# Two staging slots instead of three, and another order of the first products, in a fused attention and feed-forward kernel

## The reference, cut to what matters

```python
# 4 batches, 8 heads, 576 tokens, head size 64; d_model 512, d_ff 1536 and 2048
kv  = einsum('bhsd,bhse->bhde', k, v)
out = einsum('bhsd,bhde->bhse', q, kv)
x   = out / sqrt(mean(out*out, axis=-1) + 1e-6) * g_norm      # then tokens x 512
g   = x @ w_gate                                              # layer 1
y   = (g * sigmoid(g) * (x @ w_val)) @ w_out
h   = y @ w_in2                                               # layer 2
out = (max(h, 0) + log1p(exp(-abs(h)))) @ w_out2
```

## Time and profile before

| what | value |
|---|---|
| median of 3 runs | 906.13 us (906.01 to 907.18) |
| profiled execution | 906.13 us |
| its span, first to last instruction | 904.3 us |
| PE busy | 896.2 us (99% of the span) |
| DVE, ACT, POOL busy | 527.7, 354.8, 80.0 us |
| mean granted TensorE clock | 0.999 |

### The profile page before, as it was taken

The page is one execution under the profiler, slowest core; times in us unless marked ns, Lnnn a source line. Parts: engine busy times, 40 slices in busy tenths (PEclk is TensorE's granted clock), DMA queues, the critical chain, the costliest instruction groups (busy, mean ns, idle before and its releaser), DMA issues.

```text
span 904.3 us, 13404 instructions
## 1 busy us (share of the span) xinstructions
PE 896.2 (99%) x5146; PEld 850.1 (94%) x5146; DVE 527.7 (58%) x1009; ACT 354.8 (39%) x615; POOL 80.0 (9%) x44
## 2 busy tenths in 40 slices
PE   8999999999999999999999999999999999999998
PEld 7999999999999999999999989998998998999987
DVE  3656642453254314224234888878878878878875
ACT  5616420342034201001232754554544644644553
POOL 4635000000000000000454000000000000000000
PEclk9999999999999999999999999999999999999999
DMA  9982342133111200000243000000000000000000
GB/s 277 215 208 82 87 77 54 47 93 71 53 37 45 73 1 1 1 1 1 71 138 119 1 1 1 35 0 0 35 0 0 35 0 0 35 0 0 36 1 35
DMA packets 81129, 44.38 MB, mean 49 GB/s; under 512 B 36672, under 2 KB 73664, under 8 KB 81088
## 3 DMA queue, kind: packets, MB, share of 16 engines
q1 hardware_dynamic: 80928, 43.80, 18.2%
q10 hardware_dynamic: 160, 0.00, 0.0%
HBM read 35.52 MB, written 8.26 MB: 48 GB/s over the span
## 4 chain that ended last, share of the span: by engine, by line
PE 98%; issue 0%; DMA 0%; DVE 0%; POOL 0%; ACT 0%; ACTq 0%; POOLq 0%; SPq 0%
PE bank L655 24%; PE bank L657 24%; PE bank L656 24%; PE bank L772 7%; PE bank L773 7%; PE bank L771 7%; PE bank L595 2%; PE bank L588 1%; PE bank L663 1%; PE bank L669 0%; PE bank L561 0%; DMA q<-in_q 0%; PE bank L578 0%; PE bank L550 0%; PE bank L571 0%
## 5 line engine op out<-in xcount | busy, mean ns | idle before, releaser
L655 PE MATMUL bank<-x_hi,arena 128*128 128x384 f32 x938 | 315.1, 336 | 0.0
L657 PE MATMUL bank<-x_hi,arena 128*128 128x384 f32 x938 | 314.6, 335 | 0.0
L656 PE MATMUL bank<-x_lo,arena 128*128 128x384 f32 x938 | 314.0, 335 | 0.0
L655 PEld LDWEIGHTS bank<-x_hi,arena 128*128 128x128 f32 x938 | 176.2, 188 | 4.4
L656 PEld LDWEIGHTS bank<-x_lo,arena 128*128 128x128 f32 x938 | 176.1, 188 | 3.8
L657 PEld LDWEIGHTS bank<-x_hi,arena 128*128 128x128 f32 x938 | 176.0, 188 | 0.0
L1114 DVE TENSOR_TENSOR act_a<-act_a,bank 128x384 f32<-128x384 f32 x72 | 39.9, 554 | 228.1 <-PE bank L657 225.1
L899 ACT ACTIVATE act_a<-bank 128x384 f32<-128x384 f32 x72 | 35.3, 491 | 244.2 <-PE bank L657 240.3
L919 ACT ACTIVATE act_a<-bank 128x384 f32<-128x384 f32 x96 | 47.3, 492 | 179.1 <-PE bank L657 179.1
L773 PE MATMUL bank<-arena,g_lo 128*128 128x512 f32 x288 | 113.8, 395 | 0.0
L772 PE MATMUL bank<-arena,g_hi 128*128 128x512 f32 x288 | 113.6, 395 | 0.0
(11 more groups left out here) (90 smaller groups left out, 838.7 us busy)
## 6 DMA issues: line engine op xcount, KB each, us to landing
stage<-in_moe_w_out SPq DMA_DIRECT2D x28, 256.0 KB, 3.6
out_dram<-out_stage SPq DMA_DIRECT2D x18, 256.0 KB, 2.0
k<-in_k SPq DMA_DIRECT2D x16, 256.0 KB, 3.2
v<-in_v SPq DMA_DIRECT2D x16, 256.0 KB, 3.2
stage<-in_moe_w_in SPq DMA_DIRECT2D x16, 256.0 KB, 2.8
xy<-in_q SPq DMA_DIRECT2D x48, 72.0 KB, 3.0
stage<-in_moe_w_gate SPq DMA_DIRECT2D x12, 256.0 KB, 3.8
stage<-in_moe_w_val SPq DMA_DIRECT2D x12, 256.0 KB, 4.1
```

Source lines behind the costliest of these rows:

```text
L655: nc.tensor.matmul(ps, hi, rhs_hi, start=first, stop=False)
L656: nc.tensor.matmul(ps, hi, rhs_lo, start=False, stop=False)
L657: return nc.tensor.matmul(ps, lo, rhs_hi, start=False, stop=last)
```

## The change: what it does

- `STAGE1` goes: two slots hold the raw weights of layer 1, so load f waits for `w_ready` of step f - 2, and not f - 3. Load 2 waits for step 0 and stands behind the wait for the first transposes; load 3 stands ahead of the eight DMAs of `next_pair`, not behind them.
- The semaphores of the two layers' staging are shared.
- In a round of the first attention q times kv comes ahead of the next transpose of q, and two idle products stand in each round behind the kv product.
- The transposed x of all four rounds goes to bank 7; each transpose of x but the first waits until the previous one has been split (`xs_ready`).
- On ACT `part_high(1, "gate")` comes behind the last `first_x_high`, and the table is loaded ahead of both.
- On ACT at k = 2, `split_high(4)` comes ahead of the two roots of the late tiles.

```diff
-IDLE_PRODUCTS = (7, 2)
-STAGE1 = 3
+IDLE_PRODUCTS = (7, 2, 2)
...
-    stage1 = sb("stage1", [P, STAGE1, RAW1], F32, over="xy", shift=4 * (TOKENS * KT - STAGE1 * RAW1))
+    stage1 = sb("stage1", [P, 2, RAW1], F32, over="xy", shift=4 * (TOKENS * KT - 2 * RAW1))
...
-    qt_ps0, o_ps0, xt_ps0 = bank[3:5], bank[5:7], [bank[7], bank[1], bank[7], bank[5]]
+    qt_ps0, o_ps0, xt_ps0 = bank[3:5], bank[5:7], bank[7]
...
-    def raw_count1(f):
-        return 48 * ((f - 2) // STAGE1 + 1)
-    def raw_count2(f):
-        return 32 * (f // 2 + 1)
+    def raw_count(n):
+        return sum(48 if m < NF1 else 32 for m in range(2 + n % 2, n + 1, 2))
...
         def load_step1(f):
-            if f >= STAGE1:
-                sp.wait_ge(w_ready, low_count(f - STAGE1))
-            s = f % STAGE1
+            if f >= 2:
+                sp.wait_ge(w_ready, low_count(f - 2))
+            s = f % 2
...
         load_step1(1)
+        sp.wait_ge(qt0_done, KT)
         load_step1(2)
-        sp.wait_ge(qt0_done, KT)
+        load_step1(3)
         next_pair(1, 0)
         next_pair(1, 1)
-        load_step1(3)
         load_step1(4)
...
         def first_transpose_x(t):
             pe.wait_ge(xn0_ready, t + 1)
-            if t == 2:
-                pe.wait_ge(xs_ready, 1)
+            if t:
+                pe.wait_ge(xs_ready, t)
...
         for t in range(KT):
             first_kv_product(t)
+            idle_products(IDLE_PRODUCTS[2])
+            first_q_times_kv(t)
             if t + 1 < KT:
                 first_transpose_q(t + 1)
-            first_q_times_kv(t)
             if t:
                 first_transpose_x(t - 1)
...
-        part_high(1, "gate")
         nc.scalar.preload_act_table_set("silu_and_others")
         first_x_high(KT - 1)
+        part_high(1, "gate")
         silu(0)
...
+            if k + 2 < NF1:
+                split_high(k + 2)
             if k == 2:
                 for j in range(LATE0, NT):
                     root(-LATE0, j)
-            if k + 2 < NF1:
-                split_high(k + 2)
```

More of the change, by code:

```diff
@@ L210, in program @@
     x_back = [sem(f"x_back{n}") for n in range(3)]
-    raw_loaded1 = [sem(f"raw_loaded1_{p}") for p in range(STAGE1)]
-    raw_loaded2 = [sem(f"raw_loaded2_{p}") for p in range(2)]
+    raw_loaded = [sem(f"raw_loaded{p}") for p in range(2)]
     out_stored = sem("out_stored")
@@ L398, in load_step1 @@
                              w[:, f * P:(f + 1) * P].rearrange("(t p) n -> p t n", p=P)
-                             ).then_inc(raw_loaded1[s] if f >= 2 else part_loaded[x, f], 16)
+                             ).then_inc(raw_loaded[s] if f >= 2 else part_loaded[x, f], 16)
             sp.dma_start(stage1[:, s, 2 * KT * P:RAW1], w_out[f * P:(f + 1) * P, :]
-                         ).then_inc(raw_loaded1[s] if f >= 2 else part_loaded["out", f], 16)
+                         ).then_inc(raw_loaded[s] if f >= 2 else part_loaded["out", f], 16)
         def load_step2(f):
@@ L413, in load_step2 @@
             sp.dma_start(stage2[:, s, 0:KT * P].rearrange("p (t n) -> p t n", t=KT),
-                         w_in2[:, f * P:(f + 1) * P].rearrange("(t p) n -> p t n", p=P)).then_inc(raw_loaded2[s], 16)
-            sp.dma_start(stage2[:, s, KT * P:RAW2], w_out2[f * P:(f + 1) * P, :]).then_inc(raw_loaded2[s], 16)
+                         w_in2[:, f * P:(f + 1) * P].rearrange("(t p) n -> p t n", p=P)).then_inc(raw_loaded[s], 16)
+            sp.dma_start(stage2[:, s, KT * P:RAW2], w_out2[f * P:(f + 1) * P, :]).then_inc(raw_loaded[s], 16)
         sp.sem_inc(stage_free, 1)
@@ L484, in low_part @@
             pool.wait_ge(w_hi_ready, high_count(f, what))
-            nc.gpsimd.tensor_tensor(part1(f, 1, what), stage1[:, f % STAGE1, part_at[what]:part_at[what] + DM],
+            nc.gpsimd.tensor_tensor(part1(f, 1, what), stage1[:, f % 2, part_at[what]:part_at[what] + DM],
                                     part1(f, 0, what).bitcast(F32), ALU.subtract).then_inc(w_ready, 1)
@@ L509, in _ @@
         for f in range(2, NF1):
-            low(high_count(f), arena[:, f * SLOT1:(f + 1) * SLOT1], stage1[:, f % STAGE1, :], RAW1)
+            low(high_count(f), arena[:, f * SLOT1:(f + 1) * SLOT1], stage1[:, f % 2, :], RAW1)
         for f in range(LATE2):
@@ L567, in first_transpose_x @@
             pe.wait_ge(xn0_ready, t + 1)
-            if t == 2:
-                pe.wait_ge(xs_ready, 1)
+            if t:
+                pe.wait_ge(xs_ready, t)
             for i in range(TT):
-                last = nc.tensor.transpose(xt_ps0[t][:, i * P:(i + 1) * P], x_norm0[t % 2][:, i, :], ident[:, :])
+                last = nc.tensor.transpose(xt_ps0[:, i * P:(i + 1) * P], x_norm0[t % 2][:, i, :], ident[:, :])
             last.then_inc(xt0_done, 1)
@@ L862, in first_x_high @@
             act.wait_ge(xt0_done, t + 1)
-            nc.scalar.activation(x_hi[:, t, :], xt_ps0[t][:, 0:CH], ACT.Copy, scale=gain[:, 0:1]).then_inc(xs_hi_ready, 1)
+            nc.scalar.activation(x_hi[:, t, :], xt_ps0[:, 0:CH], ACT.Copy, scale=gain[:, 0:1]).then_inc(xs_hi_ready, 1)
         def part_high(f, what):
             act.wait_ge(part_loaded[what, f], 16)
-            nc.scalar.activation(part1(f, 0, what), stage1[:, f % STAGE1, part_at[what]:part_at[what] + DM], ACT.Copy
+            nc.scalar.activation(part1(f, 0, what), stage1[:, f % 2, part_at[what]:part_at[what] + DM], ACT.Copy
                                  ).then_inc(w_hi_ready, 1)
         def split_high(f):
-            act.wait_ge(raw_loaded1[f % STAGE1], raw_count1(f))
-            nc.scalar.activation(arena[:, f * SLOT1:f * SLOT1 + RAW1], stage1[:, f % STAGE1, :], ACT.Copy
+            act.wait_ge(raw_loaded[f % 2], raw_count(f))
+            nc.scalar.activation(arena[:, f * SLOT1:f * SLOT1 + RAW1], stage1[:, f % 2, :], ACT.Copy
                                  ).then_inc(w_hi_ready, 1)
@@ L879, in split_high2 @@
             act.wait_ge(down_done, slot_free2(f))
-            act.wait_ge(raw_loaded2[f % 2], raw_count2(f))
+            act.wait_ge(raw_loaded[f % 2], raw_count(NF1 + f))
             nc.scalar.activation(arena[:, f * SLOT2:f * SLOT2 + RAW2], stage2[:, f % 2, :], ACT.Copy
@@ L1018, in first_x_low @@
             dve.wait_ge(xs_hi_ready, t + 1)
-            nc.vector.scalar_tensor_tensor(x_lo[:, t, :], xt_ps0[t][:, 0:CH], gain[:, 0:1], x_hi[:, t, :].bitcast(F32),
+            nc.vector.scalar_tensor_tensor(x_lo[:, t, :], xt_ps0[:, 0:CH], gain[:, 0:1], x_hi[:, t, :].bitcast(F32),
                                            ALU.mult, ALU.subtract).then_inc(xs_ready, 1)
```

## The result

The changed kernel takes 913.56 us (median of 4 runs, 912.68 to 913.93) against 906.65 us (906.01 to 908.16): 6.9 us more, ratio 1.0073, interval 1.0055 to 1.009. The profiled execution took 914.56 us. Forecast were 910.8 us and at most 912.8 us. The direction and the place were right; the size was not.

What follows compares the result with a forecast made beforehand. PE, busy for 99% of the span, was taken as the bound. The sum was 906.13 + 0.9 (front shift) + 3.75 (stop at the late transposes) = 910.8 us, range 908.4 to 912.8 us.

Steps and rivals of the forecast that it cites:

- Sum on PE alone, no slack after 18 us: Whole kernel: PE is busy 99% of the span, so each us it starts later or stops comes out in full.
- Front shift, +0.9 us: First attention's rounds: uncovered transposes of q and a bank wait, less earlier q times kv; bounds +0.2 to +1.4 us.
- the order: First attention: q times kv ahead of the transposes of q, without the bank's wait, shifts the front by +0.35 us.
- the single bank: First attention, round 3: transposes of x wait for DVE's split of the previous x, to 19.3 us; one binding wait.
- within 0.05 us of when PE comes there: First attention, rounds 1 and 2: the bank's wait ends about when PE arrives; no cost was counted.
- Loads 3 and 4 and the pairs: Loads on SP: load 3 lands at 33.4 to 34.8 us; load 4, behind eight pair DMAs, lands at 40.0 us.
- The low half of step 3: POOL's half of load 3's weights, ready at 38.6 to 40.0 us, 0 to 1.3 us late for PE, absorbed.
- Roots behind split_high(4), 3.75 us: ACT waits for load 4 before the roots; step 3's val products start at 45.4, not 41.65 us; bounds 2.0 to 5.25.
- TensorE's clock: Rival, chance 0.11: idle 3.3 us near 41 us lowers PE's clock behind it; 912.0 us, or 912.5 us.
- the signs of being wrong: L602's PE wait under 1 us, matmuls behind it over 0.18 us apart, or PE waiting at an unnamed place.
- A second stop at 93 us: Rival, chance 0.09: load 11, x's trip and the turn of q delay PE 1 to 2 us; 912.3 us.
- Spread of before: Starting time of the kernel before, 906.13 us, median of three runs; 0.2%, 1.8 us, counted as distinguishable from no change.

Runs made afterwards that it cites:

- the filled gap: The changed kernel with 11 unused identity products put on PE into the idle gap ahead of the late transposes: 911.36 us, ratio 1.0047.
- the run with the slots alone: The kernel before with two slots and the new load order, roots ahead of split_high(4), old front: 907.29 us, ratio 1.0005.
- the one with the roots first: The changed kernel with one edit undone, the two roots ahead of split_high(4) on ACT again: 907.57 us, ratio 1.0005.
- the run with slots and order: The kernel before with two slots, the new load order and split_high(4) ahead of the roots, without the front edits: 913.09 us, ratio 1.0064.

## Why the prediction was wrong, step by step

- **Sum on PE alone, no slack after 18 us:** right within 0.4 us. The changed kernel's profile is 3.55 us behind that of the filled gap at the first product of step 4 (54.38 and 50.83), and 3.2 us at the end of the span (912.7 and 909.5).
- **Front shift, +0.9 us:** measured 0.85 us, or 1.0 us from the full clock of before. That the sum came so close is luck. Its parts were off in opposite directions: the order was put at +0.35 us and costs about 0.1 us (906.58 against 906.44 us at full clock), the single bank was put at one wait of about 0.5 us and costs 1.0 us. It binds in two rounds in either order; "within 0.05 us of when PE comes there" was too close to be counted as nothing.
- **Loads 3 and 4 and the pairs:** right. The low half of step 3 was put at 0 to 1.3 us late; where nothing covered it, it was 1.0 us late in the run with the slots alone. The last issue of load 4 lay 1.19 us behind its first, as before (1.18), and the landing took 5.0 us, inside 3.9 to 6.1 us. Load 4 ahead of the pairs removed the wait.
- **Roots behind split_high(4), 3.75 us:** right in mechanism and size. PE waited 3.6 us, and the run with the filled gap, where the clock plays no part, lies 3.8 us above the one with the roots first (911.36 less 907.57 us).
- **TensorE's clock: the step that failed.** The prediction gave a fall 0.11, left it out of the sum, and put it at 1.2 to 1.7 us should it come. It came in every execution of the changed kernel, and cost 2.2 us by medians (913.56 less 911.36 us), 2.9 us by the profile. The products behind the wait at 0.32 us were one of the signs of being wrong that it named. Two errors stand in it. As for the chance, I set the lack of such a gap in the trace against it, and a lack is no evidence. The Trainium skill, page "TensorE: Matmul & The Clock Gate", section "Why this matters for your kernels", warns against a gap of this length between bursts; the trace after agrees (idle 3.4 us, then a clock of 0.50). The price was taken from the small idle matmuls at the start and for their 3.35 us; the rows after show 6.8 us at the lower level, and 0.32 us for each wide product in it in place of 0.17 us. With the gap filled the changed kernel takes 911.36 us, 0.6 us above my sum, of which 0.4 us is that I started from 906.13 us.
- **A second stop at 93 us:** didn't come; PE's waits all lie ahead of 47 us.
- **Spread of before:** I took 906.13 us as what the kernel does. In the experiments 45 of 114 executions of it had a clock below 0.999, median 907.76 us, and 69 had the full clock, median 906.50 us (the 34 of 79 in an expectation above, by all that had run before it, are 39 of 91). The change's idle products remove the first kind, so part of its front cost is hidden in medians.

Read as a ladder from the full clock of before, the medians are 906.50, then 907.46 (front, +1.0), 907.57 (slots and loads, with the roots first, +0.1), 911.36 (the wait, +3.8) and 913.56 us (the clock, +2.2). Each term is the difference of two of these runs, so that they add up is no check of its own; the profile's 3.6 us of wait and 2.9 us of slow products are.

Open stays how much of the idle time can be left before the clock falls in some execution. The runs only bracket it, by the wait in the one execution profiled of each: none of five fell with 0.7 us of wait left, three of six with 2.2 us, all with 3.4 us; in the run with slots and order it fell after a wait of 2.1 us, with another of 1.2 us ahead of it, in the execution profiled.

## What to carry to other kernels

An instruction that waits for a DMA holds back all that is written behind it on its engine: what PE needs next belongs ahead of it, and moving two roots that take 0.5 us together cost 6 us here. When a forecast puts an idle time of 2 to 3 us into a dense stretch of PE, as the waits of 2.1, 2.2 and 3.4 us were here, the wait may not be the whole price; the products behind it at half rate are a case of their own, with a real chance. Where PE is sparse anyway, idle products under a wait can be free and make the time steadier (906.26 to 906.74 us in 11 executions).

## What the hardware showed unexpectedly

- A stretch of small products with waits of 0.5 to 1.1 us between them can lose the clock too: the granted clock was 0.68 from 10 to 12 us and 0.50 from 12 to 16 us, after 2 us in which PE was busy for 0.37 us. The same rounds as in the kernel before gave 0.77 and 0.50 from 8 to 12 us in the run with slots and order. About 4 of 10 executions of the kernel before have such a low mean clock, though none of those was profiled, and none of 11 with two idle products in each round.
- Two kernels with the same work differ by 1.3 us, and 1.1 us of it is a wait behind a cast of DVE that took 2.94 us in place of 0.36 us while POOL's subtraction of 3.5 us ran.
